# Sliding-window attention ahead of two MLP blocks on one core: TensorE takes attention's units in pairs, and half of a weight step is made later

## The reference

```python
scores = scale * np.matmul(q, k.transpose(0, 1, 3, 2))
keep = is_global | is_local          # n_global = 8, n_local = 96
scores = np.where(keep, scores + bias, -1e9)
a = np.exp(scores - np.max(scores, axis=-1, keepdims=True))
a = a / (np.sum(a, axis=-1, keepdims=True) + 1e-09)
attn = np.matmul(a, v)               # -> x, 1536 tokens x 512
h = x @ w_in;  x = (h * sigmoid(h)) @ w_out                  # block 1, 512 -> 2048 -> 512
h = x @ w_in2; out = (h * clip(h + 3, 0, 6) / 6) @ w_out2    # block 2
```

## Time and profile before

| | us |
|---|---|
| median of 3 runs | 601.4 (601.13 to 602.5) |
| the profiled execution, its own time | 600.91 |
| its span in the profile | 599.2 |
| PE busy | 590.4 (99%) |
| DVE, ACT, POOL busy | 373.2, 341.8, 284.8 |
| granted clock of PE | 1.00 of full speed in the mean |

### The profile page before, as it was taken

One profiled execution on the slowest core, in us unless ns is written; L12 is line 12 of the kernel. 1 busy time (PEld: TensorE's weight loads), 2 busy tenths in 40 slices (PEclk: granted clock), 3 DMA queues, 4 the chain that ended last, 5 costly groups with the idle time before them and its releaser, 6 DMA issues.

```text
span 599.2 us, 9614 instructions
## 1 busy us (share of the span) xinstructions
PE 590.4 (99%) x3429; PEld 514.0 (86%) x3429; DVE 373.2 (62%) x696; ACT 341.8 (57%) x659; POOL 284.8 (48%) x353
## 2 busy tenths in 40 slices
PE   7999999999999999999999999999999999999998
PEld 4665568999999999999999998888888988889896
DVE  7778876867655668547555775575557675554331
ACT  6999885544455657534544674454547565555441
POOL 4888995569533334369333144394333343331110
PEclk9999999999999999999999999999999999999999
DMA  8435330121221122222222122122221252121002
GB/s 349 170 134 189 108 120 25 60 105 59 91 70 59 65 71 71 71 72 71 71 72 71 36 78 71 64 70 71 71 70 36 71 188 74 56 71 36 1 1 105
DMA packets 14595, 50.05 MB, mean 84 GB/s; under 512 B 1618, under 2 KB 1874, under 8 KB 14546
## 3 DMA queue, kind: packets, MB, share of 16 engines
q1 hardware_dynamic: 14258, 48.63, 23.8%
q10 hardware_dynamic: 288, 0.79, 0.4%
HBM read 46.27 MB, written 3.15 MB: 82 GB/s over the span
## 4 chain that ended last, share of the span: by engine, by line
PE 88%; POOL 5%; DVE 3%; ACT 1%; issue 1%; DMA 0%; DVEq 0%; ACTq 0%
PE ps L967 38%; PE ps L1045 22%; PE ps L1036 14%; PE ps L1037 7%; POOL probs L304 3%; PE ps L939 2%; PE ps L914 2%; PE ps L924 2%; POOL rsume L296 1%; ACT probs L695 1%; DVE g_lo L622 1%; DVE g_f L501 0%; DVE wi_lo L476 0%; POOL x_t L341 0%; POOL x_t L336 0%
## 5 line engine op out<-in xcount | busy, mean ns | idle before, releaser
L349 POOL TENSOR_TENSOR wo_lo<-wo_raw,wo_hi 128x1024 fp32r<-128x1024 f32 x32 | 77.0, 2406 | 261.4 <-ACT wo_hi L762 255.0
L967 PE MATMUL ps<-x_hi,wi_hi 128*128 128x384 f32 x448 | 151.1, 337 | 0.5 <-DVE g_f L501 0.3
L967 PE MATMUL ps<-x_hi,wi_lo 128*128 128x384 f32 x448 | 150.0, 335 | 0.0
L967 PE MATMUL ps<-x_lo,wi_hi 128*128 128x384 f32 x448 | 150.0, 335 | 0.0
L491 DVE TENSOR_TENSOR c_sb<-ps,p_c 128x384 f32<-128x384 f32 x64 | 35.7, 557 | 159.7 <-PE ps L967 159.5
L742 ACT ACTIVATE p_c<-ps 128x384 f32<-128x384 f32 x64 | 31.5, 492 | 128.1 <-PE ps L967 127.8
L967 PEld LDWEIGHTS ps<-x_hi,wi_hi 128*128 128x128 f32 x448 | 84.1, 188 | 4.4 <-ACT u_c L742 1.0
L967 PEld LDWEIGHTS ps<-x_hi,wi_lo 128*128 128x128 f32 x448 | 84.1, 188 | 0.7
L967 PEld LDWEIGHTS ps<-x_lo,wi_hi 128*128 128x128 f32 x448 | 84.1, 188 | 0.0
L1045 PE MATMUL ps<-wo_hi,g_lo 128*128 128x512 f32 (+1 forms) x194 | 76.3, 393 | 0.0
L1045 PE MATMUL ps<-wo_lo,g_hi 128*128 128x512 f32 (+1 forms) x194 | 76.3, 393 | 0.0
(11 more groups left out here) (94 smaller groups left out, 1092.9 us busy)
## 6 DMA issues: line engine op xcount, KB each, us to landing
wi_raw<-in_w_in SPq DMA_DIRECT2D x32, 512.0 KB, 3.4
wo_raw<-in_w_out SPq DMA_DIRECT2D x32, 512.0 KB, 3.4
v_raw<-in_v SPq DMA_DIRECT2D x8, 704.0 KB, 4.1
k_raw<-in_kT SPq DMA_DIRECT2D x8, 464.0 KB, 5.0
out_y<-y_out SPq DMA_DIRECT2D x11, 256.0 KB, 4.3
q_raw<-in_qT SPq DMA_DIRECT2D x6, 384.0 KB, 5.5
q_raw<-in_qT ACTq DMA_DIRECT2D x2, 384.0 KB, 4.1
out_y<-y_out SPq DMA_DIRECT2D x2, 128.0 KB, 1.9
```

What stands on the lines that cost most here:

```text
L349: nc.gpsimd.tensor_tensor(wo_lo[:, s % 2, :], wo_raw[:, s % 2, :], wo_hi[:, s % 2, :], ALU.subtract).then_inc(wo_lo_ok, 1)
L967: mm = nc.tensor.matmul(p_bank(bank), w[:, s % 2, at], x[:, b, k, :], start=fresh and k == 0 and i == 0, stop=k == 1 and i == 2, skip_grou ...
```

## The change

PE's list for units 10 to 47 is written for two units at a time: both scores, then both transposes, of units 7 and 6 behind the later of the two, then the values of the pair before. `probs` has 8 buffers in place of 7, `probsT` 4 in place of 2, `negs` 3 in place of 2, and the waits that guard them are loosened by as much. The drain is paired too. ACT's `w_high(1, 1)` and DVE's `w_low(1, 1)` go from units 30 and 32 into the drain, `wo_high(0)` from unit 22 to unit 30, `wo_high(1)` from unit 26 into step 1. The x sums start 3 units later and end one earlier; the x halves follow. In the branch that isn't run, NLINK becomes 21. The scratch space for descriptors of dynamic DMAs is set to 4096. The core of the diff:

```diff
-LAG = 5
-DEEP = 7
+DEEP = 8
-X_SUMS = (30, 33, 35, 38, 41, 44)
-X_HIGHS = (32, 35, 40, 42, 44)
-X_LOWS = (34, 37, 41, 43, 46)
+X_SUMS = (33, 35, 37, 39, 41, 43)
+X_HIGHS = (35, 37, 40, 42, 44)
+X_LOWS = (36, 38, 41, 43, 45)
 def turned(u):
-    return SOON_TURN.get(u) if u < 10 else u - LAG
+    if u < 10:
+        return [SOON_TURN[u]] if u in SOON_TURN else []
+    return [k for k in (u - 7, u - 6) if k >= 5] if u % 2 else []
@@ DVE
-                    at_least(dve, exp_done, 2 * (u - 1))
+                    at_least(dve, exp_done, 2 * (u - 2))
@@ copy_t, DVE and ACT
-                at_least(dve, pv_done, u - 1)
+                at_least(dve, pv_done, u - 3)
@@ DVE, banded()
-                    if 20 <= u < 36 and u % 4 == 0:
+                    if u in (20, 24, 28):
                         w_low((u - 20) // 8, (u - 20) // 4 % 2)
...
                 copy_t(NU - 2)
+                copy_t(NU - 1)
+                w_low(1, 1)
                 x_low(0, T4)
-                copy_t(NU - 1)
@@ ACT, banded()
                     exps(u)
+                    if u >= 10 and u % 2 == 0:
+                        for k in turned(u + 1):
+                            if k % 3 == 0:
+                                copy_t(k)
-                    if u % 3 == 2 and u >= 8:
-                        x_copy(u // 3 - 2)
-                    if 18 <= u < 34 and u % 4 == 2:
+                    if u % 3 == 2 and u >= 11:
+                        x_copy(u // 3 - 3)
+                    if u in (18, 22, 26):
                         w_high((u - 18) // 8, (u - 18) // 4 % 2)
-                    if u in (22, 26):
-                        wo_high((u - 22) // 4)
+                    if u == 30:
+                        wo_high(0)
+                copy_t(NU - 6)
                 nc.scalar.activation(warm[:, :], three[:, :], ACT.Sigmoid)
+                x_copy(13)
                 keep(0, p1_c, 0, P1)
+                copy_t(NU - 3)
                 x_high(0, T3)
-                copy_t(NU - 3)
-                x_copy(14)
+                gated(0, 0)
+                w_high(1, 1)
                 x_high(0, T4)
@@ PE, banded()
+                for u in range(10, NU, 2):
+                    scores(u)
+                    scores(u + 1)
+                    for k in turned(u + 1):
+                        turn_probs(k)
+                    for k in (u - 8, u - 7):
+                        if k >= 4:
+                            values(k)
+                turn_probs(NU - 6)
                 turn_probs(NU - 5)
+                values(NU - 8)
+                values(NU - 7)
                 pe.wait_ge(neg_done, 2 * NU)
                 product(0, P1)
                 turn_probs(NU - 4)
+                turn_probs(NU - 3)
+                values(NU - 6)
                 values(NU - 5)
                 product(0, P2)
-                turn_probs(NU - 3)
+                turn_probs(NU - 2)
+                turn_probs(NU - 1)
                 values(NU - 4)
-                turn_probs(NU - 2)
                 values(NU - 3)
-                turn_probs(NU - 1)
```

More of the change, by code:

```diff
@@ L538, in banded @@
                         inverse(u - 1)
-                    if turned(u) is not None and turned(u) % 3:
-                        copy_t(turned(u))
-                    if 20 <= u < 36 and u % 4 == 0:
+                    for k in turned(u):
+                        if k % 3:
+                            copy_t(k)
+                    if u in (20, 24, 28):
                         w_low((u - 20) // 8, (u - 20) // 4 % 2)
@@ L565, in general @@
                 dve.sem_inc(a_score, 1)
-                NLINK = 22
+                NLINK = 21
                 with dve.Fori(0, NPAIR) as it:
@@ L598, in general @@
                         link(nc.vector.tensor_scalar(a_rel[:, :], a_rel[:, :], float(P), None, ALU.add))
-                        assert count[0] <= NLINK, count[0]
+                        assert count[0] == NLINK, count[0]
                     nc.vector.tensor_scalar(a_rel[:, :], a_rel[:, :], float(S), None, ALU.subtract).then_inc(a_link, 1)
@@ L822, in general @@
                 keep(0, p1_c, 0, P1)
-                for s in range(2):
-                    wo_high(s)
+                wo_high(0)
                 keep(0, u2_c, 0, P6)
@@ L861, in _ @@
                     y_copy(blk - 1, 2)
-                if s > 1:
-                    wo_high(s)
+                wo_high(s)
                 keep(s, u2_c, 0, P6)
@@ L972, in banded @@
             def banded():
-                for u in range(NU):
+                for u in range(10):
                     scores(u)
-                    if turned(u) is not None:
-                        turn_probs(turned(u))
-                        if turned(u):
-                            values(turned(u) - 1)
-                values(NU - 6)
+                    for k in turned(u):
+                        turn_probs(k)
+                        if k:
+                            values(k - 1)
+                for u in range(10, NU, 2):
+                    scores(u)
+                    scores(u + 1)
+                    for k in turned(u + 1):
+                        turn_probs(k)
+                    for k in (u - 8, u - 7):
+                        if k >= 4:
+                            values(k)
+                turn_probs(NU - 6)
                 turn_probs(NU - 5)
+                values(NU - 8)
+                values(NU - 7)
                 pe.wait_ge(neg_done, 2 * NU)
```

22 lines of the change are left out of this document (10 added, 12 removed).

## The result

The changed kernel takes 602.3 us, the median of 20 executions (601.23 to 603.75); the kernel before takes 601.13 (20 executions, 600.8 to 602.5). The ratio is 1.0019, with a 95% interval of 1.0011 to 1.0026: slower by 0.19%, just on the border of what can be told from no change, and not faster as predicted.

What follows compares the result with a forecast made beforehand. PE and POOL were both taken as full in attention, PE only just slower. POOL's waits -1.86, collisions -0.73 and drain +0.85 gave -1.74 us: 600.91 to 599.2, median 599.7, range 597.7 to 602.2.

Steps and rivals of the forecast that it cites:

- PE's part: In attention, a pair costs PE 3.12 us, not 3.62; 10.1 us less work, an upper end since POOL is full.
- POOL's part: In attention, fewer waits and collisions on POOL move total(47) by -2.59 us, to about 85.3.
- the two old waits: POOL's waits of 0.70 and 1.16 us for ACT in attention should both go: -1.86 us.
- the first rival: New waits eat the gain: at unit 40 ACT's x_high of T2 waits for POOL's sum; 600.3 to 602 us; chance 22%.
- The collisions with DVE's subtractions: DVE's two-input subtractions block POOL; one w_low of four leaves attention: -0.73 us.
- The drain: After attention, PE has more left when POOL finishes: P6 6.3 us behind total(47), 5.49 before; costs +0.8 us.
- The clock: Rival: with PE idle its clock falls to 1.2 GHz; 15 us over the last seven pairs, 615 us; chance 3%.
- What is moved into the drain: w_high(1, 1) on ACT and w_low(1, 1) on DVE delay nothing in the drain: 0, with 2 us of cover.
- Loads of q: PE may wait 0 to 1 us at units 24 and 30; POOL's 1.5 us to spare hide it: 0.
- The sum: Whole kernel: -1.86 - 0.73 + 0.85 = -1.74 us, from 600.91 to 599.2; predicted median 599.7.
- The signs: What the profile would show: if right, grouped records and PE waiting 0.2 to 1.2 us for norms before most pairs.
- T + 7: T is the time of total(47), POOL's last; P6 later than 7 us after it would show the forecast wrong.

Runs made afterwards that it cites:

- e10_nt_fixed: e7_nt_after with k and q loaded ahead of v, DVE's copies 40 and 41 ahead of negated(47), and P6's keep moved earlier: 593.52 us, ratio 0.9879.
- e8_fixed: e1_b22 with T2's halves a unit later, DVE's copies 40 and 41 ahead of negated(47), k and q loaded ahead of v: 600.76 us, ratio 0.9992.
- e5_fill6: The changed kernel with 6 extra matmuls, results unused, in PE's idle piece of the drain: 601.26 us, ratio 1.0002.
- e7_nt_after: The changed kernel without POOL's total; the 1e-9 is left out and DVE takes the reciprocal of the row sums themselves: 597.56 us, ratio 0.9953.
- e4_pairs: The changed kernel with the weights' work back in attention; pairs, buffers and x units as changed: 603.63 us, ratio 1.0047.
- e1_b22: The changed kernel with ACT's and DVE's halves of x quarter B22 moved from units 44 and 45 into the drain: 600.67 us, ratio 0.9996.

## Why the prediction was wrong, by its own steps

- **PE's part** (3.12 us for a pair in place of 3.62) was right: 3.11 and 3.61. That this is no gain by itself because POOL is full was right too: it took e10_nt_fixed to see it as time.
- **POOL's part**, -2.59, came as -1.37, so it falls short by 1.2. Its terms: the two old waits went as forecast, but three new ones of 1.42 us came, so -0.44 in place of -1.86, and that is the term that was mis-sized. The largest, 0.64 at 75.71, is the coupling that the first rival described at unit 40: ACT's `x_high` of T2 waited 1.95 us for POOL's sum (73.80) and held back the exponentials; its price was 0.5. The collisions with DVE's subtractions gave -0.8 (seven with 5.5 us, before nine with 6.3, by what POOL's records exceed their usual length), for a term of -0.73. That e8_fixed takes 65.15 us for the stretch, 0.03 from the forecast, does not bear the terms out: B22's halves are out of it there and waits of 0.81 us are left.
- **The drain**, "+0.8", came as +3.20, and this is the step that failed. It followed PE's own work and POOL's norms and did not follow DVE: `turn_probs(k)` also waits for the copy of unit k-2, and those copies stand behind two `negated` and `x_low(B22)`. At full clock (e5_fill6) the drain costs 7.12 - 5.49 = 1.63, against 0.8, and the fall of the clock adds 1.6. With the copies ahead of `negated(47)` and B22 out of the way (e8_fixed) it costs 6.36 - 5.49 = 0.87: what the step did follow, it followed rightly.
- **The clock** was given 3% as a rival and was priced for seven pairs in a row, 15 us. In the profiled execution it fell behind one single gap, for less than 6 us of time, and cost 1.6 us (e5_fill6); nine of 20 executions have the mean of 0.997 that goes with it, and their median is 1.9 us above the others'. The argument against it, full clock where PE is busy only 6.79 of 10 us, did not carry over to one long gap. The Trainium skill (TensorE: Matmul & The Clock Gate, Part 4: PE-mode transpose) says that transposes do not count as busy in the same way for the clock gate. Transposes and values stand on both sides of the gap here, which fits; but no run changed them alone, and in e10_nt_fixed the clock is 1.00 all through such work, where no wait of PE is over 1.3 us.
- **What is moved into the drain**, 0, held in the profile of the changed kernel: P6 to step 1 takes 6.79 there, as before (6.82). Its cover is thin: where ACT's and DVE's work comes later in relation to P6, as in e8_fixed, 1.0 us more passes until step 1.
- **Loads of q**: PE's waits of 0 to 1 us, hidden, were 1.4 us in three places. They were hidden (POOL does not wait for them), and with POOL relieved became 3.9.
- **The sum** itself takes +0.85 for a drain that was worked out as 6.3 - 5.49 = 0.81; that changes nothing.
- **The signs** of being wrong that are there: POOL waiting for ACT, a clock under 1.00, and P6 later than T + 7 (T + 8.69). Of those of being right, the grouped records are there, but PE was to wait for norms before most pairs and waits for them once; its idle time stands before the scores, for negated maxima (4.1 us).
- That the change was no gain at all, 1.2 us slower by the medians where 1.7 faster was forecast, is thus two things, in the profiled execution 1.2 us less from attention and 2.4 more lost in the drain.

Left open: why the clock falls in nine of 20 executions of the changed kernel, in five of seven of e7_nt_after and in all six of e4_pairs. One execution of each has a trace: in the first and the last the gap is 2.08 us and the clock falls behind it, in e7_nt_after it is 2.02 and the clock stays. How long the gap was in the others is not on record.

## What to carry over

When two engines are both full, grouping work on one of them only builds up the other's queue; relieve the second engine first, then look again at every wait that its fullness had hidden. When an order is made coarser, walk through every buffer between the engines, those that the change leaves alone too, and ask in which engine's list the release stands and behind what. Price a new gap on TensorE twice: its own length, and, in case the clock falls, the work behind it at half the clock. And when a stretch comes out at the number that was forecast, see whether it did so by the terms of the forecast.

## What the runs showed of the hardware

- In the traces of the changed kernel and of e4_pairs the granted clock fell (to 0.50 and 0.55 in a stretch of 2 us) behind a single idle time of 2.08 us in the midst of transposes and values; behind 2.02 us in that of e7_nt_after, and 1.27 us in that of e1_b22, it did not. The mean of 0.997 that goes with such a fall shows in nine of 20, six of six, five of seven and none of 11 executions of these four. With six useless matmuls in the gap it shows in none of 12.
- Such a matmul of 128x128 by 128 columns in float32 took 0.23 us of PE's time in a row of 14 and 0.27 in a row of six.
- The Trainium skill (GPSIMD Engine Reference, 8. Key points) says that GpSimd shares its SBUF interfaces with VectorE and contends with VectorE's instructions that have two SBUF inputs. The traces agree and give the size: POOL's addition over 128x2 takes 0.92 in place of 0.19 us beside such an instruction, and seven meetings cost 5.5 us in the changed kernel.
- A tiny instruction is not tiny in its queue: an addition over 128x2 on DVE in front of the reciprocal that reads it cost 0.20 us a unit, 2.5 times what the reciprocal takes.
